# First block in pairs of feature chunks, its down product with tokens as rows and both sides split, PSUM sums left open; scores in three banks, rings of three, y in DRAM

## What is computed

```python
scores = scale * np.matmul(q, k.transpose(0, 1, 3, 2))       # per head 576 x 576
kth = np.partition(scores, -32, axis=-1)[..., -32:-31]
scores = np.where(scores >= kth, scores, -1000000000.0)
attn = softmax(scores)                                       # with 1e-9 added to the sum
x = np.matmul(attn, v)                                       # 1152 x 512 after joining heads
h = x @ w_in                                                 # 512 -> 2048
g = np.maximum(h, 0.0) + alpha * np.minimum(h, 0.0)
y = g @ w_out                                                # 2048 -> 512
out = ((y @ w_a) * (y @ w_b)) @ w_o                          # 512 -> 1536 -> 512
```

## Time and profile before

| | us |
|---|---|
| median of 3 runs | 703.82 (703.82 to 704.25) |
| the profiled execution | 702.61 |
| its span, first to last instruction | 700.8 |
| TensorE busy | 624.0 (89%) |
| VectorE busy | 428.0 (61%) |
| ScalarE busy | 334.2 (48%) |
| GpSimd busy | 250.4 (36%) |

### The profile page before, as it was taken

How to read it: one execution, slowest core, us unless ns; L and a number is a source line. 1 busy time by engine, 2 the same in 40 slices (tenths; PEclk the granted TensorE clock), 3 DMA queues, 4 the chain that set the end, 5 groups by cost and what they waited for, 6 DMA issues and landing times.

```text
span 700.8 us, 11978 instructions
## 1 busy us (share of the span) xinstructions
PE 624.0 (89%) x4700; PEld 549.9 (78%) x4700; DVE 428.0 (61%) x859; ACT 334.2 (48%) x740; POOL 250.4 (36%) x345
## 2 busy tenths in 40 slices
PE   3266778878899998999989989999999999999997
PEld 1154667767888787887878879889999999999996
DVE  6999999999989889898898103433222211121112
ACT  3666656667764677645776326533221311131113
POOL 2665566347772377723777128400000000000000
PEclk9967999999999999999999989999999999999999
DMA  9521500001011100100000003441100100010001
GB/s 310 155 91 36 220 1 16 2 16 35 19 35 35 49 1 2 61 1 1 1 1 2 1 1 94 135 148 66 56 0 1 46 1 0 1 46 0 1 1 45
DMA packets 18392, 30.40 MB, mean 43 GB/s; under 512 B 3104, under 2 KB 7456, under 8 KB 18336
## 3 DMA queue, kind: packets, MB, share of 16 engines
q1 hardware_dynamic: 18336, 29.64, 13.4%
HBM read 27.27 MB, written 2.36 MB: 42 GB/s over the span
## 4 chain that ended last, share of the span: by engine, by line
PE 63%; DVE 21%; POOL 5%; issue 5%; ACT 4%; DMA 0%; SPq 0%; ACTq 0%; POOLq 0%; DVEq 0%
PE m_ps L784 12%; DVE top L607 12%; DVE work L617 9%; PE sc_ps L820 7%; PE sc_ps L818 7%; PE sc_ps L819 7%; PE m_ps L770 4%; PE m_ps L774 3%; PE m_ps L772 3%; POOL p_sb L384 2%; PE o_ps L728 2%; PE sc_ps L688 2%; PE t_ps L702 1%; PE t_ps L832 1%; PE o_ps L833 1%
## 5 line engine op out<-in xcount | busy, mean ns | idle before, releaser
L607 DVE MAX8 top<-work 128x8 f32<-128x576 f32 x216 | 155.0, 773 | 0.0
L784 PE MATMUL m_ps<-g_sb,wout 128*128 128x256 f32 (+1 forms) x640 | 135.1, 364 | 0.0
L384 POOL TENSOR_TENSOR p_sb<-s_sb,p_sb 128x576 f32<-128x576 f32 x72 | 101.3, 1417 | 73.3 <-ACT p_sb L428 73.3
L784 PEld LDWEIGHTS m_ps<-g_sb,wout 128*128 128x128 f32 x640 | 110.4, 192 | 18.4 <-issue 5.9
L649 DVE TENSOR_TENSOR ab<-sc_ps,a_sb 128x384 f32<-128x384 f32 x36 | 20.1, 558 | 147.1 <-PE sc_ps L820 147.1
L617 DVE MATCH_REPLACE8 work<-top,work 128x576 f32<-128x576 f32 x144 | 107.9, 772 | 0.0
L728 PE MATMUL o_ps<-v_sb,pT 128*64 128x64 f32 x576 | 45.4, 239 | 40.7 <-ACT pR L446 40.5
L770 PE MATMUL m_ps<-xT_parts,win_hi 128*128 128x256 f32 x256 | 77.1, 301 | 3.1 <-issue 3.1
L728 PEld LDWEIGHTS o_ps<-v_sb,pT 128*64 128x64 f32 x576 | 40.7, 151 | 48.4 <-issue 48.0
L772 PE MATMUL m_ps<-xT_parts,win_hi 128*128 128x256 f32 x256 | 73.4, 287 | 0.0
L774 PE MATMUL m_ps<-xT_parts,win_lo 128*128 128x256 f32 x256 | 73.3, 286 | 0.0
(11 more groups left out here) (96 smaller groups left out, 1415.5 us busy)
## 6 DMA issues: line engine op xcount, KB each, us to landing
stage<-in_w_in SPq DMA_DIRECT2D x8, 512.0 KB, 4.2
wout<-in_w_out SPq DMA_DIRECT2D x1, 4096.0 KB, 15.4
k_sb<-in_kT SPq DMA_DIRECT2D x12, 288.0 KB, 4.0
stage<-in_w_a SPq DMA_DIRECT2D x8, 384.0 KB, 3.2
stage<-in_w_b SPq DMA_DIRECT2D x8, 384.0 KB, 3.2
stage<-in_w_o SPq DMA_DIRECT2D x6, 512.0 KB, 3.6
out<-o_sb SPq DMA_DIRECT2D x9, 256.0 KB, 2.2
q_sb<-in_qT SPq DMA_DIRECT2D x8, 256.0 KB, 2.7
```

The costliest lines, as they stand in the source:

```text
L384: nc.gpsimd.tensor_tensor(p_sb[:, row, :], s_sb[:, row, :], p_sb[:, row, :], ALU.subtract).then_inc(masked, 1)
L607: largest = nc.vector.max(top32[:, row, 8 * r:8 * r + 8], work[:, c, :] if r else s_sb[:, row, :])
L784: done = nc.tensor.matmul(m_ps[:, bank, 0:n], wout[:, f, d * P:(d + 1) * P], g_sb[:, f, 0:n], start=(f == 0), stop=(f == FC1 - 1))
```

## The change

Attention:
- The scores of a pair lie side by side in 1152 columns of three banks (they were in four banks of 288 columns each), cut at bank borders into parts of 256 and 320 columns. The middle bank is shared by both heads, and the fourth part waits for the first. ScalarE copies both heads in one instruction.
- k_sb, q_sb, v_sb and s_sb are rings of three pairs, loaded pair by pair. v is laid out by the host with its remainder rows placed in blocks, so vr_sb and pR are gone, and ScalarE copies the second head's transposes and the shared remainder in one instruction of 640 columns.
- `times_v` of pair i-1 runs in step i, behind the first turn. Steps go to 36.

First block: it runs in chunks n of two features (256 columns of PSUM each, one bank), one chunk a step, from step 5 on. `fill(i)` gives the chunk for up and the chunk before it for down. The down product has g as weights (tokens as rows) and w_out as moving operand (512 columns), both split, and its sums stay open in banks ACC and ACC+1 over all 8 chunks. GpSimd makes g_lo, ScalarE g_hi, and w_out is split at the start like w_in. The split tile's up product has three matmuls of 128 columns a k chunk, like the others; VectorE's additions are gone. The rows of y go by `evict_y` to ytok and by DMA to y_dram. The last group has two buffers for each stage, and the low parts of w_a and w_b are made beside it, in place of a stage.

Second block: y is loaded 384 tokens at a time, transposed on TensorE (`turn_y`) and split, three transposes for each of 4 chunks and pass; for passes 1 and 2 these stand in rounds 5 to 8 of the pass before. The eight chunks of the second half of w_a and w_b are loaded after the last up product and the six of w_o after the last down product. The operands of w_o's products are unchanged in number and shape.

```diff
-SLOTS = 4
-FIRST_UP = 4
+FP1 = FC1 // 2
+RING = 3
+FIRST_UP = PAIRS + 1
+W2_ORDER = [0, 1, 2, 3, 4, 5, 6, 7, 16, 17, 8, 9, 10, 11, 18, 12, 13, 14, 19, 15, 20, 21]
+W2_BESIDE = {0: [17, 8, 9], 1: [10, 11], 2: [18, 12], 3: [13, 14], 4: [19, 15], 6: [20], 8: [21]}
...
+        def fill(i):
+            if not FIRST_UP <= i < FIRST_UP + LAST * FP1:
+                return None, None
+            g, n = divmod(i - FIRST_UP, FP1)
+            up = (Group(g), n)
+            if n:
+                return up, (Group(g), n - 1)
+            return up, (Group(g - 1), FP1 - 1) if g else None
...
 # SyncE, at the end of its queue
+            sp.wait_ge(u_full, Group(LAST).up_use(FP1 - 1) + 1)
+            sp.wait_ge(y_saved[1], 16 * 2)
+            sp.wait_ge(y_saved[2], 16 * 2)
+            load_y(0)
+            for c in range(8, WAB):
+                load_w2(c)
+            sp.wait_ge(down_done, GROUPS * FP1)
+            for c in range(WAB, WAB + WO):
+                load_w2(c)
+            save_y(Group(LAST))
...
 # GpSimd, step(i)
+                if chain is not None:
+                    bound(chain)
+                if output is not None and output.hp == PAIRS - 1:
+                    denominator(output)
+                if chain is not None:
+                    mask(chain, 0)
+                if first_turn(i - 1) is not None:
+                    lo_of_x(first_turn(i - 1), 0)
+                    if up[0].n > P:
+                        lo_of_x(up[0], 1)
+                if finished is not None and finished.hp == PAIRS - 1:
+                    normalise(finished)
+                if down is not None:
+                    lo_of_g(*down)
+                if chain is not None:
+                    mask(chain, 1)
+                if w_in_chunk(i) is not None:
+                    lo_of_w_in(w_in_chunk(i))
+                if w_out_chunk(i) is not None:
+                    lo_of_w_out(w_out_chunk(i))
+                if up is not None:
+                    slope_and_sum(*up)
...
 # ScalarE
+            def copy_scores(pair):
+                act.wait_ge(scored, pair.number + 1)
+                if pair.number >= RING:
+                    act.wait_ge(masked, 2 * (pair.number - RING + 1))
+                nc.scalar.activation(s_sb[:, pair.slot].rearrange("p c n -> p (c n)"), flat[:, SC:SC + 2 * S],
+                                     ACT.Copy).then_inc(copied, 2)
...
+            def step(i):
+                score, chain, output, finished = pair(i + 3), pair(i + 1), pair(i), pair(i - 1)
+                up, down = fill(i)
+                opens = up is not None and up[1] == 0
+                if output is not None:
+                    evict_turned(output, 0)
+                if first_turn(i - 1) is not None:
+                    evict_x_turn(first_turn(i - 1), 0)
+                if chain is not None:
+                    relu(chain, 0)
+                if finished is not None and finished.hp % 2:
+                    evict_output(finished)
+                if opens and up[0].n > P:
+                    evict_x_turn(up[0], 1)
+                if chain is not None:
+                    relu(chain, 1)
+                if down is not None:
+                    hi_of_g(*down)
+                if chain is not None:
+                    exp(chain, 0)
+                if score is not None:
+                    copy_scores(score)
+                if up is not None and not opens:
+                    halves_of_h(*up)
+                if output is not None:
+                    evict_turned(output, 1)
+                if chain is not None:
+                    exp(chain, 1)
...
+                if up is not None and up[1] == 1 and up[0].g:
+                    evict_y(Group(up[0].g - 1))
+                if opens:
+                    halves_of_h(*up)
...
 # VectorE, before the second block
+            for c in range(8):
+                lo_of_w2(c)
+            for k, bank in enumerate((U, 1, 2, 3)):
+                lo_of_y(0, k, bank)
+            lo_of_w2(WAB)
+            dve.wait_ge(y_saved[LAST], 16 * 2)
...
 # TensorE
+            def down(group, n, t):
+                _, _, g_hi, g_lo = buffers(group, n)
+                rows = slice(t * P, (t + 1) * P)
+                if t == 0:
+                    pe.wait_ge(glo_done, group.seq(n) + 1)
+                    if group.g == 0:
+                        pe.wait_ge(olo_done, n + 1)
+                    elif n == 0:
+                        pe.wait_ge(acc_out, group.tiles_before)
+                for half in range(2):
+                    f = 2 * n + half
+                    nc.tensor.matmul(ps[:, ACC + t, :], g_hi[:, half, rows], wout_hi[:, f, :], start=(f == 0), stop=False)
+                    nc.tensor.matmul(ps[:, ACC + t, :], g_hi[:, half, rows], wout_lo[:, f, :], start=False, stop=False)
+                    done = nc.tensor.matmul(ps[:, ACC + t, :], g_lo[:, half, rows], wout_hi[:, f, :],
+                                            start=False, stop=(f == FC1 - 1))
+                if t == len(group.tiles) - 1:
+                    done.then_inc(down_done, 1)
+
+            def step(i):
+                score_of, output, finished = pair(i + 3), pair(i), pair(i - 1)
+                go_up, go_down = fill(i)
+                opens = go_up is not None and go_up[1] == 0
+                if output is not None:
+                    turn(output, 0)
+                if finished is not None:
+                    times_v(finished)
+                if go_up is not None and not opens:
+                    up(*go_up, 0)
+                if opens and go_up[0].n > P:
+                    turn_x(go_up[0], 1)
+                if score_of is not None:
+                    score(score_of)
+                if go_up is not None and not opens:
+                    up(*go_up, 1)
+                if output is not None:
+                    turn(output, 1)
+                if opens:
+                    up(*go_up, 0)
+                if go_down is not None:
+                    down(*go_down, 0)
+                if opens:
+                    up(*go_up, 1)
+                if go_down is not None and go_down[0].n > P:
+                    down(*go_down, 1)
+                if first_turn(i) is not None:
+                    turn_x(first_turn(i), 0)
```

More of the change, by code:

```diff
@@ L106, in attention_ffn @@
[L106 to L112, removed]
@@ new lines, in next_kq, with save_y, load_w2 @@
+            def next_kq(number):
+                if number < N_PAIRS:
+                    sp.wait_ge(scored, number - RING + 1)
+                    load_kq(pair(number))
+            def save_y(group):
+                for t in range(len(group.tiles)):
+                    sp.wait_ge(acc_out, group.tiles_before + t + 1)
+                    sp.dma_start(y_dram[group.row + t * P:group.row + (t + 1) * P, :], ytok[:, t, :])\
+                      .then_inc(y_saved[group.g], 16)
+            def load_w2(c):
+                raw, _, _ = w2_chunk(c)
+                if c >= WAB:
+                    f = 2 * (c - WAB)
@@ L408, in _ @@
+            for i in range(FIRST_STEP, N_PAIRS + 1):
+                if i == FIRST_UP:
+                    pool.wait_ge(alpha_in, 16)
+                step(i)
+            lo_of_g(Group(LAST - 1), FP1 - 1)
+            group = Group(LAST)
+            lo_of_x(group, 0)
+            lo_of_x(group, 1)
+            for n in range(FP1):
+                slope_and_sum(group, n)
+                if n:
+                    lo_of_g(group, n - 1)
+            lo_of_g(group, FP1 - 1)
         @block.scalar
@@ new lines, in hi_of_g, with evict_y @@
+            def hi_of_g(group, n):
+                pos, _, g_hi, _ = buffers(group, n)
+                act.wait_ge(sum_done, group.seq(n) + 1)
+                if group.g == LAST and n >= 2:
+                    act.wait_ge(down_done, group.seq(n) - 1)
+                elif group.seq(n) and not group.odd(n):
+                    act.wait_ge(down_done, group.seq(n))
+                nc.scalar.activation(g_hi[:, :, 0:group.n], pos[:, :, 0:group.n], ACT.Copy).then_inc(ghi_done, 1)
+            def evict_y(group):
+                act.wait_ge(down_done, group.seq(FP1 - 1) + 1)
+                if group.g < LAST:
+                    act.wait_ge(xlo_done, Group(group.g + 1).tiles_after)
+                for t in range(len(group.tiles)):
+                    nc.scalar.activation(ytok[:, t, :], ps[:, ACC + t, :], ACT.Copy).then_inc(acc_out, 1)
@@ L693, in turn @@
+                done.then_inc(scored, 1)
             def turn(pair, c):
-                row = 2 * pair.par + c
+                both = p_sb[:, pair.par].rearrange("p c n -> p (c n)")
                 pe.wait_ge(expd, pair.u + c + 1)
@@ new lines, in _, with turn_y @@
+            group, before = Group(LAST), Group(LAST - 1)
+            for t in range(2):
+                down(before, FP1 - 1, t)
+            turn_x(group, 1)
+            for n in range(FP1):
+                for half in range(2):
```

(14 more changed lines are left out.)

962 lines of the change are left out of this document (453 added, 509 removed).

## The result

The changed kernel takes 735.39 us (median of 4, 734.61 to 737.36) against 703.82 (700.72 to 704.25): ratio 1.046, 95% interval 1.043 to 1.050. It is 4.6% slower, where 699.3 was forecast. The profiled execution has a span of 732.8 us (before 700.8, forecast 696.3) and a mean clock of 0.932 (before 0.969).

A forecast was written before the change was run, and what follows sets the result against it. VectorE's top-32 bounds before 160 us, TensorE after. Second block's start 453.8 + 225.9 + 3.4 + 5.7 + 3.1 = 691.9, with 4.4 of copies and stores span 696.3, scaled to 699.3 us; range 677 to 714.

The forecast's parts named there:

- I cost GpSimd's low parts ... at nothing: the spare s_sb slot covers 4.7 us: Early steps: low parts of w_in and w_out, 2.5 us each, add no time; TensorE begins step 13 at 147.6.
- Group: 75.9 + 2.9 + 3.9 = 82.7.: Eight steps: TensorE work 75.9 us, opening wait 2.9, second step's wait for acc_out 3.9; 88.2 before.
- To the last group ... 8.8 later ... 1.6 for the first g.: From step 13 through the last group: up starts 8.8 us after 390.0, one 1.6 wait, second block at 453.8.
- Second block: Three passes 225.9 us, y transposes 3.4, wait for the y save 5.7, half clock behind it 3.1.
- The down product: First block: 12 matmuls of 512 columns at 0.231 us each, 2.77 a step, 0.68 less than before.
- 128 columns of f32r: Split tile's up products in the early steps: taken as 0.06 us a matmul, half the time of 256 columns.
- Rival 3: Split tile's 128-column f32r matmuls take the fp32 instruction's time, 0.216 us: 704 us; chance 0.08.
- Rival 1: Waits are covered: TensorE keeps 9.64 us through the groups and the y save lands in time: 677 us; chance 0.26.
- The one on the slower side: Every down product waits for its own g low part, 1.0 us in each of 24 steps: 722 us; chance 0.20.
- Step starts 9.4 apart inside a group and about 12 and 13 at its first two: Expected sign in the groups: step spacing in us, longer at the opening and second steps.
- VectorE waiting little before 160 us: Expected sign in the early part: VectorE waits little there, and some 0.7 us a step after.
- the signs of being wrong: Steps near 11 us, second block beginning after 465, or no TensorE idle stretch in the second block.

The follow-up runs named there:

- the best version: Changed kernel with weights' low parts a step later, y saved and evicted earlier, w_in parts early, x's low part first and the last group reordered: 677.40 us.
- The last edit: Against the 688.34 us kernel, in the last group x's second tile turned before the last down product, g's low part before slopes and sum: 677.40 us.
- the three edits together: Changed kernel with low parts of the weights a step later, last saves of y ahead of w_o's loads, and y evicted earlier: 696.10 us.

## Why the prediction was wrong

Two parts of the span account for it, counted from VectorE's last pair (378.27 in the kernel before, 389.63 after, 353.42 in the best version): the change lost 11.4 us up to there and 20.6 behind it; the best version gains 24.9 and loses 1.1.

**"I cost GpSimd's low parts ... at nothing: the spare s_sb slot covers 4.7 us"** is the step that failed, 24.4 of the 36.5 us. I priced the instruction (2.5; measured 2.37) and named a cover of 4.7 without a working, but did not price its wait, nor the queue behind it: the low part waited for a high part that ScalarE makes last in its step, with the next pair's bounds behind it. A slot absorbs one delay; this one came back each step. The delay was 2.9 us a step (12.5 against 9.64); moving the low part by a step took 18.9 off in all. Of the other 5.5 (step 13 at 153.05 instead of 147.6), 1.7 are already there at step 5 (72.22, where eight steps of 9.64 back from 147.6 give 70.5); the rest is volume, as the steps of 11.1 to 11.6 us show. Moving w_in took 3.1 off by step 13, though the total did not gain.

**"Group: 75.9 + 2.9 + 3.9 = 82.7."** Measured 87.1, 86.0 and 79.6, the last against 77.0. The second failed step is here, 10.3 us over three groups. The waits were placed rightly: the opening wait for x was 1.82 in each group where 2.9 was charged, and the wait for acc_out 4.36, 3.41 and 3.41 for 3.9; evicting y early brought the first group to 82.2. What was missing: the half clock behind that wait, 1.8 us in the first two groups (15.85 less 9.67 less 4.36 in the first), which I had charged in two other places on the strength of the earlier trace rows but not here; and a steady step of 9.67 instead of 9.36. Of that 0.31 the scores are 0.21: cut into four parts of 256 and 320 columns they take 1.38 a step (290.01 to 291.39), where I had kept the 1.17 of four parts of 288, the same number of columns. The ups (3.15 for 3.06) and the down product (2.84 for 2.77) are most of the rest.

**"To the last group ... 8.8 later ... 1.6 for the first g."** The up began 11.2 after the turn of x, 2.4 late, and the second block 3.1 late in all: a mis-sized term. The last edit shows that most of these waits were order.

**Second block.** Right in its mechanism and to 1.3 us in its sum: wait 6.02 (forecast 5.7), w_o issued first, slow matmuls behind it (2.2 for 3.1), period 6.27. With the save first the wait shrinks to 1.57.

**The down product.** Right: starts 0.23 apart where the clock is full. Removing four of the twelve took 0.90 off a step, 0.225 each.

**128 columns of f32r.** Measured about 0.11 a matmul (99.75 to 101.24), not 0.06; but with the early steps set by the loop between ScalarE and GpSimd it decided nothing. Rival 3 had its premise in part and not its price.

**Rivals.** Rival 1 did not come: the waits were not covered. The one on the slower side named the right kind of mechanism, in-order queues between ScalarE and GpSimd, at the wrong place: it looked at g's low part in the groups, and the loop sat in the weights' low parts before them. "Step starts 9.4 apart inside a group and about 12 and 13 at its first two" held but for 9.67 and up to 15.9. "VectorE waiting little before 160 us" did not hold: four waits for scores (6.7 us) and two for a denominator (6.3) stand there. Of the signs of being wrong, the early steps ran at 12.5 us, above the 11 that was named, and the second block began at 491.6, after 465.

## What to carry to other kernels

An instruction on a side engine has three prices: its time, the wait it starts with, and what stands behind it in its queue. When a step's operand comes from another engine's last work of the same step, take the operand of the step before; the same work then cost 16 us less here. Find the engine whose work is conserved (here VectorE, 9.64 a pair) and value each edit by what it takes off that engine's idle time, then look for gaps on TensorE in the stretches where it has no work, for several of them cost more than their length: slow matmuls stood behind them.

## What the runs showed of the hardware

GpSimd and VectorE held each other up in the last group, where both add or subtract tensors in SBUF. In the changed kernel, VectorE's low part of w_a took 1.07 when it started first and 1.66 when it started behind a GpSimd instruction, and GpSimd's sum of 512 columns took 1.88 against 1.27 alone:

```profile
442.30 1.07 DVE L688 TENSOR_TENSOR wab<-wab_raw,wab 128x768 fp32r<-128x768 f32 x1 [31.94 <-ACT wab L609]
445.96 1.66 DVE L688 TENSOR_TENSOR wab<-wab_raw,wab 128x768 fp32r<-128x768 f32 x1 [2.59 <-ACT wab L609]
```

```profile
442.65 1.88 POOL L421 TENSOR_TENSOR pos_neg<-pos_neg 128x512 f32<-128x512 f32 x1
...
445.53 1.27 POOL L421 TENSOR_TENSOR pos_neg<-pos_neg 128x512 f32<-128x512 f32 x1
446.76 1.98 POOL L427 TENSOR_TENSOR g_parts<-pos_neg,g_parts 128x512 fp32r<-128x512 f32 x1
```

VectorE's instruction ends at 443.37; GpSimd's, had it begun only then, would end at 443.37 + 1.27 = 444.64, and it ended at 444.53. VectorE's second instruction, had it begun only when GpSimd's sum ended (445.53 + 1.27 = 446.80), would end at 447.87, and it ended at 447.62. By the Trainium skill (SBUF — State Buffer, SBUF: two separate sides) the port pair that the two share is an exclusive lock for the whole instruction, also for a VectorE operation with two SBUF inputs beside a GpSimd operation that reads SBUF; the trace agrees to 0.1 us in the first case and 0.25 in the second.

The clock did not follow the length of a wait alone. Behind waits of 1.84 and 1.83 us for x, before the second and third group's first up product of the three edits together, it was 1.00 and 0.88 over the opening step, with the same instructions.

MAX8 and MATCH_REPLACE8 took 745 and 743 ns in the changed kernel against 773 and 772 before, though GpSimd did more beside them. The pace of a pair was the same all the same, 9.66 us (8.46 to 18.12) and 9.65 (8.07 to 17.72). No run here says why.
